# Attention and two gated MLPs: value loads cut to the rows that are read

## The chip, the cores and the metric

The program runs on one core of one Trainium2 chip. A core has TensorE (PE in the profile, its weight loads PEld), VectorE (DVE), ScalarE (ACT), GpSimd (POOL), SyncE (SP), and 16 DMA engines that move data between HBM and SBUF. The metric is the device time of one execution in microseconds, median of several runs.

## The reference

```python
q, k, v: (4 batches, 8 heads, 576 tokens, 64)          # attention
q_d, k_d, v_d = mean over groups of 4 tokens            # 144 pooled tokens
out_d = softmax(scale * q_d @ k_d.T) @ v_d              # pooled attention
out_up = repeat(out_d, 4, axis=tokens)
mask = |i - j| < 4                                      # local attention: a band of 7 keys
out_local = softmax(where(mask, scale * q @ k.T, -1e9)) @ v
x = (out_up + out_local) as (2304 tokens, 512)
x = (sigmoid(x @ w_gate) * (x @ w_val)) @ w_out         # first MLP, inner width 1536
h = x @ w_in;  x = (h * sigmoid(1.702 * h)) @ w_out     # second MLP, inner width 2048
```

All in float32.

## The kernel before

The 32 pairs of batch and head are worked through as 16 units of two heads. After the units the two MLPs run as a long row of 128x128 by 128x384 matmuls (lines 662 to 664, 653 and 808 to 810).

**Local attention of a unit.** The 576 queries are cut into 12 windows of 48. A window needs 56 keys (four more on each side). `weigh(u)` (L615) multiplies, for each window and head, the turned probabilities `p_t` by the values `vw`: 57 rows, the 56 keys and one row that carries a small constant for the sum of probabilities. Head 0 stands in partitions 0 to 56, head 1 in partitions 64 to 120; rows 57 to 63 and 121 to 127 of `vw` are loaded and never read. One row of `vw` is 12 windows of 65 numbers, 3120 bytes.

**Pooled attention of a unit.** `sum_values(u)` (L556) adds values over groups of four tokens with five matmuls of 128 tokens each (`vt`, 5 chunks of 128 columns, two heads side by side). 576 tokens fill four chunks and 64 rows of the fifth; the other 64 rows of the fifth come from HBM as zeros. One row of `vt` is 2560 bytes. `sum_values_1` (L567) is the same for unit 1 in another bank.

**The loads.** All are issued by SP in one program order. `load_q` and `load_k` have four buffers, `load_vt` and `load_vw` two. `load_vw(u)` (L348) waits until `weigh(u - 2)` is over, `load_vt(u)` (L343) until the pooled scores of unit u - 2 are made. Ahead of the loop stand, in this order, q and k of unit 0, `vt` 0, q and k of 1, `vw` 0, `vt` 1, q and k of 2, `vw` 1, q and k of 3. In the loop (L453) step i issues `vw` i + 2, q and k of i + 6, `vt` i + 4, and in ten of the steps a half of an MLP weight block (`load_in_half`, `load_out_half`), 256 KB. Each load raises its semaphore by 16 when it has landed.

**PE's order.** In the loop (L876) PE runs for unit i: `weigh(i)`, the mask of i + 2, `turn(i + 1)`, `score(i + 2)`, `turn_out(i)`, `weigh_pooled(i)`, `sum_values(i + 2)`, `score_pooled(i + 2)`, `turn_pooled(i + 1)`. Nothing is reordered at run time: an instruction that waits holds all behind it. Between `weigh(14)` and `weigh(15)` the first products of the MLP stand (L889 to L894).

**Ahead of it all** DVE clears constants and pads; its last one, `p_t`, raises `zeroed` (L1587), for which PE waits ahead of `sum_values(0)`, and the casts of `picks` and `mask` come after.

Of the kernel before, what the change touches and what calls it, by code (L numbers as in the profile page):

```python
# [14 lines left out]
B, H, S, D = 4, 8, 576, 64  # L15
FACTOR = 4
P = 128
# [10 lines left out]
KW = QW + 2 * PAD  # L28
# [3 lines left out]
HK = 64  # L32
SD = S // FACTOR
SD1 = SD - P
VT = 5
HQ = SD // 2
VC = D + 1
SCALE = 1.0 / D ** 0.5
# [92 lines left out]
def attention_mlp_kernel(nc, q_t, k_t, v_win, v_tok, w_gate_val, w_out1, w_in2, w_out2, out):  # L131
    with ExitStack() as ctx:
        top = [16512]

        def place(name, shape, dtype=F32, at=None):
            size = 2 if dtype == BF16 else 4
            for s in shape[1:]:
                size *= s
            where = top[0] if at is None else at
            if at is None:  # L140
                top[0] += (size + 31) // 32 * 32
            return nc.alloc_sbuf_tensor_at(name, shape, dtype, offset=where)
# [4 lines left out]
        def sems(name, n):  # L147
            return [sem(f"{name}{i}") for i in range(n)]
# [16 lines left out]
        w = [place(f"w{i}", [P, 2, NP, WG], F32R) for i in range(2)]  # L165
# [17 lines left out]
        vw = [place(f"vw{i}", [P, NWIN, VC]) for i in range(2)]  # L183
        vt = [place(f"vt{i}", [P, VT, P]) for i in range(2)]
        e = place("e", [P, PAIRS, 2, HK])
        p_t = place("p_t", [P, NWIN, HK])
        o_tok = place("o_tok", [P, PAIRS, 2, D])
        pd = [place(f"pd{i}", [HQ, 4, SD]) for i in range(2)]
        pd_t = place("pd_t", [P, 2, 2, SD])
# [55 lines left out]
        vw_loaded = sems("vw_loaded", 2)  # L245
        vt_loaded = sems("vt_loaded", 2)
# [76 lines left out]
        def _(sp):  # L323
# [19 lines left out]
            def load_vt(u):  # L343
                if u >= 2:
                    sp.wait_ge(scored_d, u - 1)
                sp.dma_start(vt[u % 2][:, :, :].rearrange("p j d -> p (j d)"), v_tok[u]).then_inc(vt_loaded[u % 2], 16)

            def load_vw(u):  # L348
                if u >= 2:
                    sp.wait_ge(weighed, u - 1)  # L350
                sp.dma_start(vw[u % 2][:, :, :].rearrange("p w d -> p (w d)"), v_win[u]).then_inc(vw_loaded[u % 2], 16)

            def load_in(b):

# [89 lines left out]

            load_qk(0)
            load_vt(0)
            load_qk(1)
            load_vw(0)
            load_vt(1)
            load_qk(2)  # L450
            load_vw(1)
            load_qk(3)
            for i in range(-2, UNITS - 2):  # L453
                if i >= 0:
                    load_vw(i + 2)
                if i + 6 < UNITS:
                    load_qk(i + 6)
                if i + 4 < UNITS:
                    load_vt(i + 4)
                if i in (-1, 0):  # L460
                    load_in_half(0, i + 1)
                if i in (1, 2):
                    load_in_half(1, i - 1)
                if i in (3, 4):
                    load_out_half(0, i - 3)
                if i in (8, 9):
                    if i == 8:
                        sp.wait_ge(wa_ready, 1)
                        sp.wait_ge(wsum_ready, 1)
                    load_in_half(2, i - 8)  # L470
                if i in (10, 11):
                    load_out_half(1, i - 10)
# [61 lines left out]
        def _(pe):  # L534
# [20 lines left out]

            def sum_values(u):  # L556

                pe.wait_ge(vt_loaded[u % 2], 16 * (u // 2) + 16)
                if u >= 2:
                    pe.wait_ge(exped_d, u)  # L560
                    pe.wait_ge(v_summed, u)
                for j in (0, 2, 1, 3, 4):
                    bank, at = divmod(j // 2 * 64, P)
                    pe.matmul(d_ps[at:at + 64, bank, VS_AT:VS_AT + P], fours[:, j % 2, :], vt[u % 2][:, j, :],
                              start=(j % 2 == 0), stop=(j % 2 == 1 or j == VT - 1))

            def sum_values_1():  # L567

                pe.wait_ge(vt_loaded[1], 16)
                for j in (0, 2, 1, 3, 4):  # L570
                    c, at = divmod(j // 2 * 64, P)
                    mm = pe.matmul(t_ps[at:at + 64, 1, VS1_AT + c * P:VS1_AT + (c + 1) * P], fours[:, j % 2, :], vt[1][:, j, :],
                                   start=(j % 2 == 0), stop=(j % 2 == 1 or j == VT - 1))
                mm.then_inc(sums_turned, 1)

            def score_pooled(u):
# [4 lines left out]
                for half in range(2):  # L581
                    for h in range(2):
                        rows = slice(h * D, (h + 1) * D)
                        mm = pe.matmul(d_ps[0:HQ, h, half * SD:(half + 1) * SD],
                                       qkd[u % 2][rows, 0, half * HQ:(half + 1) * HQ], qkd[u % 2][rows, 1, :],
                                       start=True, stop=True)
# [13 lines left out]
            def turn_pooled(u):  # L600
# [6 lines left out]
                for c, keys in enumerate((slice(0, P), slice(P, SD))):  # L607
                    for h in range(2):
                        for half in range(2):
                            at = c * SD + half * HQ  # L610
                            mm = pe.transpose(t_ps[0:keys.stop - keys.start, h, at:at + HQ],
                                              pd[u % 2][:, 2 * h + half, keys], ident[0:HQ, 0:HQ])
                mm.then_inc(turned_d, 1)

            def weigh(u):  # L615

                pe.wait_ge(copied, u + 1)
                pe.wait_ge(vw_loaded[u % 2], 16 * (u // 2) + 16)
                if u >= 1:
                    pe.wait_ge(added, u)  # L620
                for pair in range(PAIRS):
                    for par in range(2):
                        w = 2 * pair + par
                        for h in range(2):
                            rows = slice(HK * h, HK * h + KW + 1)
                            mm = pe.matmul(o_ps[HK * par:HK * (par + 1), h, pair * VC:(pair + 1) * VC],  # L626
                                           p_t[rows, w, :], vw[u % 2][rows, w, :], start=True, stop=True)
                mm.then_inc(weighed, 1)
# [226 lines left out]
            pe.wait_ge(fours_step, 3)  # L855
            pe.wait_ge(zeroed, 1)
            sum_values(0)
            score_pooled(0)
            masks(1)
            score(1)  # L860
            pe.wait_ge(ident_ready, 1)
            turn(0)
            sum_values_1()
            score_pooled(1)
            weigh(0)
            masks(2)
            turn_pooled(0)
            score(2)
            turn_out(0)
            turn(1)  # L870
            sum_values(2)
            weigh_pooled(0)
            score_pooled(2)
            turn_pooled(1)
            last = UNITS - 1
            for i in range(1, UNITS - 2):  # L876
                weigh(i)
                masks(i + 2)
                turn(i + 1)
                score(i + 2)  # L880
                turn_out(i)
                weigh_pooled(i)
                sum_values(i + 2)
                score_pooled(i + 2)
                turn_pooled(i + 1)
            weigh(last - 1)
            turn(last)
            pe.wait_ge(shifted, UNITS)
# [624 lines left out]
        def _(dve):  # L1513
            vec = nc.vector
# [67 lines left out]
                vec.memset(qk[slot][:, 1, PAD + S:S + 2 * PAD], 0.0)  # L1582
            vec.memset(e[:, :, :, KW:KW + 1], 1.0)
            vec.memset(e[:, :, :, KW + 1:HK], 0.0)
            vec.memset(d_ps[:, 1, VS_AT:VS_AT + P], 0.0)
            vec.memset(t_ps[:, 1, VS1_AT:VS1_AT + 2 * P], 0.0)
            vec.memset(p_t[:, :, QW:HK], 1.0).then_inc(zeroed, 1)  # L1587
# [3 lines left out]
            for half in range(2):  # L1591
                rows = slice(HK * half, HK * half + HK)
# [4 lines left out]
            for half in range(2):  # L1597
                rows = slice(HK * half, HK * half + QW)
# [801 lines left out]
```

## Time and profile before

| | us |
|---|---|
| median of 3 runs | 871.63 (871.37 to 872.4) |
| the profiled execution, its own time | 872.51 |
| its span in the profile | 870.8 |
| PE busy in it | 857.5 |
| DVE, ACT, POOL busy | 624.1, 487.0, 589.2 |
| last `weigh` starts | 109.67 |

The span runs from the first instruction to the last; the 1.7 us around it belong to start and end of the execution. In the timeline a row is: start in us, duration in us, engine, line, operation, tiles (output <- inputs), shapes and how many instructions were merged; in brackets the idle time ahead of it and what ended that. A line such as L626 is a line of the kernel printed above. The attention is about the first eighth of the span, the MLPs all the rest.

### The profile page before, as it was taken

Reading aid. Unit: us, or ns where it says so; the run is one execution under the profiler, and the core shown is the slowest. Engines: PE = TensorE matmul, PEld = TensorE weight load, DVE = VectorE, ACT = ScalarE, POOL = GpSimd, SP = SyncE. Lnnn points to the kernel's source line nnn. Section 1 sums busy time; section 2 is a strip of 40 time slices with the busy share of each in tenths; the row PEclk is TensorE's granted clock in tenths of the full one; section 3 lists DMA queues with packets and bytes.
Section 4 is the critical chain, followed back from the end, with each engine's and each line's share of the span. In section 5 each row is a group of like instructions: output and inputs, shape, how many; then the busy total and the mean of one; then the engine's idle time right before and its main releaser. Section 6 shows DMA issues by size and latency. Waiting matters only on the chain.

```text
span 870.8 us, 18384 instructions
## 1 busy us (share of the span) xinstructions
PE 857.5 (98%) x6638; PEld 832.2 (96%) x6638; DVE 624.1 (72%) x1140; ACT 487.0 (56%) x1083; POOL 589.2 (68%) x471
## 2 busy tenths in 40 slices
PE   8989999999999999999999999999999999999998
PEld 6878899999999999999999999999999999999998
DVE  5767645555658685967676877777888778878777
ACT  5778754545536364645354646654676466556652
POOL 6688788888758648785457776763668644846523
PEclk9999999999999999999999999999999999999999
DMA  9877466685955787838588825345246751636432
GB/s 329 264 211 218 166 242 237 223 342 204 382 172 192 294 287 292 301 109 285 210 274 305 285 91 205 97 147 195 67 174 218 266 183 59 218 123 230 171 120 73
DMA packets 77369, 184.26 MB, mean 212 GB/s; under 512 B 5856, under 2 KB 31456, under 8 KB 74464
## 3 DMA queue, kind: packets, MB, share of 16 engines
q1 hardware_dynamic: 77280, 183.10, 60.2%
q8 instruction: 53, 0.87, 0.4%
q14 instruction: 36, 0.29, 0.1%
HBM read 141.66 MB, written 41.42 MB: 210 GB/s over the span
## 4 chain that ended last, share of the span: by engine, by line
PE 94%; issue 2%; DVE 1%; ACT 1%; POOL 1%; DMA 1%; SPq 0%; ACTq 0%; DVEq 0%
PE o_ps L808 10%; PE o_ps L809 10%; PE o_ps L810 10%; PE d_ps L662 7%; PE d_ps L664 7%; PE d_ps L663 7%; PE s_ps L662 6%; PE o_ps L653 6%; PE s_ps L664 6%; PE s_ps L663 6%; PE t_ps L662 3%; PE t_ps L663 3%; PE t_ps L664 3%; PE o_ps L626 2%; PE t_ps L597 1%
## 5 line engine op out<-in xcount | busy, mean ns | idle before, releaser
L808 PE MATMUL o_ps<-g_hi,v 128*128 128x384 f32 x504 | 169.6, 337 | 0.6 <-DVE att L1773 0.5
L809 PE MATMUL o_ps<-g_lo,v 128*128 128x384 f32 x504 | 169.4, 336 | 0.0
L810 PE MATMUL o_ps<-g_hi,v 128*128 128x384 f32 x504 | 169.4, 336 | 0.0
L1773 DVE TENSOR_TENSOR att<-o_ps,att 128x384 f32<-128x384 f32 x212 | 118.1, 557 | 56.4 <-PE o_ps L810 53.8
L2123 POOL TENSOR_TENSOR v<-v_f,v 128x512 fp32r<-128x512 f32 x72 | 95.0, 1340 | 56.2 <-ACT v L1076 56.2
L2123 POOL TENSOR_TENSOR v<-raw,v 128x512 fp32r<-128x512 f32 x54 | 70.9, 1312 | 89.8 <-ACT v L1069 77.2
L662 PE MATMUL d_ps<-xs_hi,w 128*128 128x384 f32 x360 | 121.0, 336 | 2.0 <-issue 1.2
L664 PE MATMUL d_ps<-xs_hi,w 128*128 128x384 f32 x360 | 120.5, 335 | 0.0
L663 PE MATMUL d_ps<-xs_lo,w 128*128 128x384 f32 x360 | 120.4, 335 | 0.0
L662 PE MATMUL s_ps<-xs_hi,w 128*128 128x384 f32 x300 | 101.2, 337 | 1.3 <-POOL xs_lo L2153 1.3
L664 PE MATMUL s_ps<-xs_hi,w 128*128 128x384 f32 x300 | 100.5, 335 | 0.0
L663 PE MATMUL s_ps<-xs_lo,w 128*128 128x384 f32 x300 | 100.4, 335 | 0.0
L808 PEld LDWEIGHTS o_ps<-g_hi,v 128*128 128x128 f32 x504 | 94.6, 188 | 1.8 <-issue 1.8
L809 PEld LDWEIGHTS o_ps<-g_lo,v 128*128 128x128 f32 x504 | 94.8, 188 | 0.0
L810 PEld LDWEIGHTS o_ps<-g_hi,v 128*128 128x128 f32 x504 | 94.6, 188 | 0.0
L1191 ACT CAST g_hi<-t_ps 128x384 fp32r<-128x384 f32 x96 | 46.2, 481 | 84.8 <-DVE t_ps L1701 45.0
L662 PEld LDWEIGHTS d_ps<-xs_hi,w 128*128 128x128 f32 x360 | 67.6, 188 | 3.9 <-issue 3.4
L1645 DVE TENSOR_TENSOR g_lo<-g_f,g_hi 128x384 fp32r<-128x384 f32 x68 | 62.1, 914 | 7.9 <-ACT g_hi L1174 7.9
L663 PEld LDWEIGHTS d_ps<-xs_lo,w 128*128 128x128 f32 x360 | 67.6, 188 | 0.0
L664 PEld LDWEIGHTS d_ps<-xs_hi,w 128*128 128x128 f32 x360 | 67.6, 188 | 0.0
L2153 POOL TENSOR_TENSOR xs_lo<-xs_sum,xs_hi 128x768 fp32r<-128x768 f32 x24 | 46.9, 1965 | 26.1 <-ACT xs_hi L1040 26.0
L662 PE MATMUL t_ps<-xs_hi,w 128*128 128x384 f32 x180 | 60.4, 335 | 0.0
(186 smaller groups left out, 2099.6 us busy)
## 6 DMA issues: line engine op xcount, KB each, us to landing
w<-w_split SPq DMA_DIRECT2D x48, 768.0 KB, 7.0
w<-w_split SPq DMA_DIRECT2D x48, 512.0 KB, 7.8
w<-w_split SPq DMA_DIRECT2D x96, 256.0 KB, 5.3
w_split<-w SPq DMA_DIRECT2D x12, 1792.0 KB, 6.7
raw<-in_w_out_dram SPq DMA_DIRECT2D x36, 512.0 KB, 4.5
w_split<-job_w SPq DMA_DIRECT2D x8, 1792.0 KB, 7.7
vw<-in_v_win_dram SPq DMA_DIRECT2D x16, 390.0 KB, 4.6
raw<-in_w_gate_val_dram SPq DMA_DIRECT2D x24, 256.0 KB, 3.3
```

The source lines that it names most:

```text
L653: mm = pe.matmul(bank, a, b, start=(i == 0), stop=(i == len(steps) - 1))
L662: pe.matmul(bank, wh[:, cols], xh[:, c, :], start=(start and c == 0), stop=False, skip_group_check=True)
L663: pe.matmul(bank, wh[:, cols], xl[:, c, :], start=False, stop=False, skip_group_check=True)
L664: mm = pe.matmul(bank, wl[:, cols], xh[:, c, :], start=False, stop=(c == 1), skip_group_check=True)
L808: pe.matmul(bank, vh, gh, start=(start and k == c), stop=False, skip_group_check=True)
L809: pe.matmul(bank, vh, gl, start=False, stop=False, skip_group_check=True)
L810: mm = pe.matmul(bank, vl, gh, start=False, stop=(k == c + 1), skip_group_check=True)
L1191: nc.scalar.copy(g_hi[k % 2][:, t, :], bank[LAST[k] % 2]).then_inc(thi_ready[t], 1)
L1645: vec.tensor_tensor(g_lo[k % 2][:, PIECE[n], :], gated_at(k, n, bank), g_hi[k % 2][:, PIECE[n], :], ALU.subtract).then_inc(g_ready[n], 1)
L1773: vec.tensor_tensor(part, value, part, ALU.add).then_inc(y_added, 1)
L2123: gp.tensor_tensor(v_all[:, :, 1, v_part, :], source, v_all[:, :, 0, v_part, :], ALU.subtract).then_inc(vp_ready, 1)
L2153: gp.tensor_tensor(xs_lo[at][:, :, :], source, xs_hi[at][:, :, :], ALU.subtract).then_inc(x_ready, 1)
```

## The change

The load of `vw` becomes two, of rows 0 to 56 and 64 to 120. The load of `vt` becomes two: four chunks of all 128 rows (2048 bytes a row), and the fifth chunk of 64 rows (512 bytes a row). The other half of the fifth chunk is cleared once by DVE in both buffers. The semaphores now rise by 32 for each unit, and the waits count so.

```diff
+V_END = S - (VT - 1) * P
...
             def load_vt(u):
                 if u >= 2:
                     sp.wait_ge(scored_d, u - 1)
-                sp.dma_start(vt[u % 2][:, :, :].rearrange("p j d -> p (j d)"), v_tok[u]).then_inc(vt_loaded[u % 2], 16)
+                sp.dma_start(vt[u % 2][:, 0:VT - 1, :].rearrange("p j d -> p (j d)"), v_tok[u][:, 0:(VT - 1) * P]).then_inc(vt_loaded[u % 2], 16)
+                sp.dma_start(vt[u % 2][0:V_END, VT - 1, :], v_tok[u][0:V_END, (VT - 1) * P:VT * P]).then_inc(vt_loaded[u % 2], 16)
 
             def load_vw(u):
                 if u >= 2:
                     sp.wait_ge(weighed, u - 1)
-                sp.dma_start(vw[u % 2][:, :, :].rearrange("p w d -> p (w d)"), v_win[u]).then_inc(vw_loaded[u % 2], 16)
+                for h in range(2):
+                    rows = slice(HK * h, HK * h + KW + 1)
+                    sp.dma_start(vw[u % 2][rows, :, :].rearrange("p w d -> p (w d)"), v_win[u][rows, :]).then_inc(vw_loaded[u % 2], 16)
...
-                pe.wait_ge(vt_loaded[u % 2], 16 * (u // 2) + 16)
+                pe.wait_ge(vt_loaded[u % 2], 32 * (u // 2) + 32)
...
-                pe.wait_ge(vt_loaded[1], 16)
+                pe.wait_ge(vt_loaded[1], 32)
...
-                pe.wait_ge(vw_loaded[u % 2], 16 * (u // 2) + 16)
+                pe.wait_ge(vw_loaded[u % 2], 32 * (u // 2) + 32)
...
             vec.memset(e[:, :, :, KW + 1:HK], 0.0)
+            for i in range(2):
+                vec.memset(vt[i][V_END:P, VT - 1, :], 0.0)
             vec.memset(d_ps[:, 1, VS_AT:VS_AT + P], 0.0)
```

SP's queue ahead of the loop, before. The number after a tile's name is a buffer, and rows x columns stand last.

```order
L346 DMA vt_87<-in_v_tok_dram 128x640
L331 DMA qk_82<-in_q_t_dram 128x576
L337 DMA qk_82<-in_k_t_dram 128x576
L351 DMA vw_85<-in_v_win_dram 128x780
L346 DMA vt_88<-in_v_tok_dram 128x640
```

The same place now:

```order
L347 DMA vt_87<-in_v_tok_dram 128x512
L348 DMA vt_87<-in_v_tok_dram 64x128
L332 DMA qk_82<-in_q_t_dram 128x576
L338 DMA qk_82<-in_k_t_dram 128x576
L355 DMA vw_85<-in_v_win_dram 57x780 x2
L347 DMA vt_88<-in_v_tok_dram 128x512
L348 DMA vt_88<-in_v_tok_dram 64x128
```

Nothing changes places; `vt` and `vw` are now two issues each, in the places of the one. In the kernel before every load has 128 rows; the two of `vw` now have 57 and the second of `vt` has 64.

## Rows read from the trace of the kernel before

**Rows 1.** The page, busy time of each engine over the span.

```profile
PE 857.5 (98%) x6638; PEld 832.2 (96%) x6638; DVE 624.1 (72%) x1140; ACT 487.0 (56%) x1083; POOL 589.2 (68%) x471
```

**Rows 2.** DMA packets, and all issues: tiles, queue, count, KB each, us to landing.

```profile
DMA packets 77369, 184.26 MB, mean 212 GB/s; under 512 B 5856, under 2 KB 31456, under 8 KB 74464
...
w<-w_split SPq DMA_DIRECT2D x48, 768.0 KB, 7.0
w<-w_split SPq DMA_DIRECT2D x48, 512.0 KB, 7.8
w<-w_split SPq DMA_DIRECT2D x96, 256.0 KB, 5.3
w_split<-w SPq DMA_DIRECT2D x12, 1792.0 KB, 6.7
raw<-in_w_out_dram SPq DMA_DIRECT2D x36, 512.0 KB, 4.5
w_split<-job_w SPq DMA_DIRECT2D x8, 1792.0 KB, 7.7
vw<-in_v_win_dram SPq DMA_DIRECT2D x16, 390.0 KB, 4.6
raw<-in_w_gate_val_dram SPq DMA_DIRECT2D x24, 256.0 KB, 3.3
vt<-in_v_tok_dram SPq DMA_DIRECT2D x16, 320.0 KB, 4.5
qk<-in_q_t_dram SPq DMA_DIRECT2D x16, 288.0 KB, 3.5
qk<-in_k_t_dram SPq DMA_DIRECT2D x16, 288.0 KB, 4.0
job_raw<-in_w_in_dram SPq DMA_DIRECT2D x8, 512.0 KB, 8.8
v_f<-in_w_out_dram SPq DMA_DIRECT2D x12, 256.0 KB, 7.0
out_dram<-att SPq DMA_DIRECT2D x2, 1536.0 KB, 12.6
out_dram<-att SPq DMA_DIRECT2D x8, 192.0 KB, 1.9
```

**Rows 3.** Windows: us, busy of each engine (instructions), granted clock, DMA share, GB/s.

```profile
7.50:10.90 3.40, 3.40 (x65) 2.50 (x62) 0.75 (x1) 1.07 (x5) 1.81 (x2) 0.54 1.03 398
44.00:50.00 6.00, 3.70 (x115) 2.96 (x114) 2.10 (x4) 3.87 (x14) 3.86 (x5) 1.00 0.66 215
```

**Rows 4.** Timeline of PE in the attention, some of its rows.

```profile
6.92 1.26 PE L564 MATMUL d_ps<-vt,fours 128*64 128x128 f32 x10 [1.65 <-DMA vt<-in_v_tok_dram]
...
17.28 0.87 PE L564 MATMUL d_ps<-vt,fours 128*64 128x128 f32 x10
...
49.59 0.41 PE L551 MATMUL s_ps<-qk 64*48 64x56 f32 x13 [2.30 <-issue]
...
59.37 0.93 PE L626 MATMUL o_ps<-vw,p_t 57*64 57x65 f32 x48
...
65.41 0.93 PE L626 MATMUL o_ps<-vw,p_t 57*64 57x65 f32 x48
...
71.45 0.93 PE L626 MATMUL o_ps<-vw,p_t 57*64 57x65 f32 x48
...
101.83 0.93 PE L626 MATMUL o_ps<-vw,p_t 57*64 57x65 f32 x48
...
109.67 0.93 PE L626 MATMUL o_ps<-vw,p_t 57*64 57x65 f32 x48
```

**Rows 5.** Timeline of SP's queue: the first load, and one of `vw`.

```profile
0.80 0.39 SPq L331 DMA_DIRECT2D qk<-in_q_t_dram  x1
...
60.36 0.33 SPq L351 DMA_DIRECT2D vw<-in_v_win_dram  x1
```

**Rows 6.** Timeline of DVE at the start: a clear of 128x128.

```profile
1.52 0.17 DVE L1585 MEMSET d_ps<- 128x128 f32 x1
```

## The prediction

> **What bounds the kernel now.** I read the busy line of the page first, then TensorE's timeline in the attention, then the DMA parts and the windows. The busy line has PE at 857.5 us of a span of 870.8 [rows 1], so any time in which PE stands longer is added to the end nearly one for one. In the attention one unit follows the other at the pace of PE: `weigh` starts at 59.37, 65.41 and 71.45, 6.04 us a unit, with no idle time ahead of it, and the two last start at 101.83 and 109.67, with MLP products between them [rows 4]. Values are waited for in one place, at the start: `sum_values(0)` stands 1.65 us for `vt` [rows 4]. The loads run far ahead: `vw` of unit 9 is issued at 60.36 [rows 5] and read at 71.45 [rows 4], and such a load lands 4.6 us after its issue [rows 2]. So there is little to win from fewer bytes, and about 11 us of lead to lose per unit before PE notices. The question is what the new shapes do to the DMA engines.
>
> **The bytes.** `vw` goes from 128 to 114 rows, 390 to 347 KB; `vt` from 320 to 288 KB. That is 75 of 1286 KB for a unit (q and k are 576 of it) [rows 2], 6%.
>
> **How a load is spread, the term that decides.** All issues of the kernel sum to 366 (the 15 kinds), and there are 5856 packets under 512 B [rows 2]; 5856 / 366 is 16.0. No data row of before is that short (the shortest piece is 1 KB), so these are the completion marks, one for each of 16 engines: each load, always of 128 rows, is split over all 16, 8 rows each. No load of another count is in the trace. 57 is 3 x 19. If a load is split into equal shares over at most 16 engines, which is all that rows 2 show, 57 rows go over 3 engines (or one), 19 rows each; 64 rows go over 16. If the shares may be unequal, 57 rows go four to an engine, over 15. I take the equal split over 3, and the same 3 for both halves.
> The Trainium skill, "DMA: Bandwidth & Descriptors", section "Why a DMA increments its semaphore by 16 and not by 1", has it as a rule: the number of engines is the largest up to 16 that divides the row counts of both sides, with 100 rows on 10 engines as an example, and always the lowest-numbered ones. No row of before can test it, since 128 gives 16.
>
> **What the three engines then carry.** When all are busy (share 1.03) they move 398 GB/s, 24.9 GB/s each [rows 3]. At that rate, for an engine among the three:
> - q and k of a unit: 16 rows of 2304 bytes, 1.48 us
> - `vt`: 8 rows of 2048 and 4 of 512 bytes, 0.74 us (before, 8 rows of 2560: 0.82)
> - `vw`: 2 x 19 rows of 3120 bytes, 118.6 KB, 4.76 us (before, 8 rows: 1.00)
> - a half block of MLP weights, 256 KB over 16: 0.66 us, in ten of the units.
> Sum 6.98 us a unit, 7.64 with a half block; before it was 3.30 and 3.96. Both new ones are above PE's 6.04. The three engines become the bound of the attention, and since the lead of 11 us is finite, PE stands at `weigh` in nearly each unit.
>
> **The sum.** Engine 0 to the end of `vw` 14, whose loads are issued behind q, k and `vt` of all 16 units and all ten half blocks: 16 x 1.48 = 23.7, 16 x 0.74 = 11.8, 15 x 4.76 = 71.4, 10 x 0.66 = 6.6, together 113.5 us. It is not idle on the way: at first it has a backlog, and later each `weigh` waits for it while the next `vw` is already queued. Ahead of that stands the first issue at 0.80 [rows 5], and the fixed part of a load, 3.5 us to landing of an early q less 0.74 us of moving [rows 2], 2.8 us. So `vw` 14 lands at 117.1. `weigh(14)` started at 101.83: 15.3 us later. From there to `weigh(15)` PE has 7.8 us of other work and `vw` 15 comes 4.8 us behind `vw` 14, hidden. That is the lower figure, at the best rate. Packets in a less tidy queue, and the start, where the engines are not yet full, cost some per cent: with 3% on 113.5 it is 18.7. I take 17.5. The profiled execution took 872.51, 0.9 over the median of 871.63; on it the sum gives 890.0, on the median 889.1. I say 889.5, 2.1% slower.
> Bounds for the price of a row of `vw` on one engine: 125 ns from the full rate [rows 3]; from above, (4.6 - 2.8) us / 8 rows = 0.23 us, from the median landing with all that stands ahead of it in the queue [rows 2]. By that a unit has 8.7 us for `vw` alone and `vw` 14 comes 59 us later still. A queue that never empties is the case of [rows 3], so I stay near the first.
>
> **The same at the start.** `vt` 2 is behind `vw` 0 and `vw` 1 on the three engines: 5 pairs of q and k 7.4, three `vt` 2.2, two `vw` 9.5, sum 19.1 us, landing at 22.7. PE wants it at 17.28 [rows 4], so `sum_values(2)` stands some 5 us. This is not added to the sum: the engines work through it, and it is the first part of the same 17.5.
>
> **The small parts.** SP issues 32 loads more. An issue takes 0.33 us in the loop [rows 5], two more per 6.04 us, and SP waits there most of the time: 0. Ahead of the loop four more issues stand, 0.4 us each [rows 5], before q and k of unit 3; behind the DMA backlog: 0 (at most 1.6 us, if there were none). DVE's two clears of 64x128 take about 0.17 us each, as the 128x128 one [rows 6], ahead of the casts that PE's first scores wait for. It costs nothing as long as PE waits for `vt` 0 until 6.92 with 1.65 us to spare [rows 4], else 0.34 us. PE's matmuls are the same.
>
> **The rivals.**
> - Unequal shares, or other engines for each load in turn. Then an engine carries no more than the 8 rows of `vw` for a unit that it carried before, on average, so 3.2 to 3.9 us, under 6.04, and the lead hides all: 871.6, at most a few tenths less for the 32 KB taken from `vt` 0. For it speaks only that rows 2 show nothing but 128 rows.
> - The clock comes on top. PE ran at half (mean 0.54) in 7.50 to 10.90 [rows 3] after it had stood 1.65 us, having run for few us before. There five-chunk sums take 1.26 us and not 0.87 [rows 4]; by 1.45 a unit takes 8.8 us, above 7.6, and PE itself becomes the bound where that happens. If half of 14 units run so, 7 x (8.8 - 7.3) = 10 us more: 900. Against it: at 49.59 PE had stood 2.30 us [rows 4], and the clock of that stretch is 1.00 [rows 3]; the waits I expect are 0.9 to 1.6 us. One early fall behind the 5 us stand is likely, and hidden by the engines' backlog.
> - One engine, the other equal split: 114 x 0.125 + 2.2 = 16.5 us a unit, 1030 us or so.
> - Faster. With all 16 engines in use, `vt` 0 could come early enough that PE doesn't stand at 6.92 and keeps its clock. That is 1.65 us, and about 1.1 us for the 3.4 us at half clock (3.4 - 3.4 / 1.45): 868.9. It decides only if `vt` 0 lands 1.6 us earlier; ahead of and in it 864 KB stand in place of 896, 0.1 us at 398 GB/s. So hardly.
>
> **How the numbers follow.** Three engines, 879 to 900: 0.74. With the clock or dearer packets, above that: 0.09, and one engine 0.01. Unequal shares, no change: 0.12. Faster by the start: 0.04. No change means within 0.2%, 1.7 us, about what a measurement of this kernel can tell. Slower has the first three, 0.84. The range from 879 to 906 holds the three-engine case with the bottom at 6 us of regained time (PE's later idle, shorter packets than I took) and most of the clock's; it leaves out 0.2.
>
> **What would show it.** Right: packets in the two halves of `vw` from 3 engines, so a mean DMA share in the attention that falls while PE stands; `vw` landing 7 us or more after its issue; waits of PE for a DMA at L630 (the former L626) of about 1 us in some ten units; `weigh` 7.0 to 7.7 us apart; a stand of about 5 us at the third `sum_values`; the last `weigh` near 127; the MLPs as long as before. Wrong: `weigh` still 6.04 us apart and `vw` landing in under 5 us, which is the split over all 16; or PE rows of 1.26 us for five chunks in the middle of the attention, which is the clock.

## The result: 3.3% slower

| | before | after |
|---|---|---|
| median of 6 runs, us | 870.96 | 899.51 |
| lowest and highest | 870.29, 872.40 | 896.39, 903.17 |
| profiled execution, its own time | 872.51 | 896.39 |
| span in the profile | 870.8 | 894.6 |

The ratio after to before is 1.0328, with a 95% interval of 1.0311 to 1.0345. I had forecast 889.5 us, 2.1% slower, with 879 to 906 as the range. The direction and the mechanism came out; the loss is 28.5 us between the medians and not 18. The profiled execution is the fastest of the six, 23.9 us over the one of before; what follows explains those 23.9.

**All of it is in the attention.** Windows of PE for the MLPs alone, from 17.3 us behind the start of the last `weigh` to the end; first the kernel before, then the one after. The columns are those of [rows 3].

```profile
127.00:870.80 743.80, 736.87 (x4218) 732.13 (x4216) 542.17 (x972) 399.12 (x810) 493.90 (x359) 1.00 0.59 208
```

```profile
150.70:894.60 743.90, 737.10 (x4218) 732.49 (x4217) 540.84 (x972) 399.73 (x810) 494.55 (x359) 1.00 0.59 208
```

The same work takes 743.8 and 743.9 us. So the 23.8 us of the span lie ahead of it.

**Three engines.** The page after, the line of the DMA packets, against the first of [rows 2]:

```profile
DMA packets 78265, 183.04 MB, mean 205 GB/s; under 512 B 5952, under 2 KB 32576, under 8 KB 75360
```

Packets under 512 B are the completion marks (the shortest data rows are 512 B). Of the 366 loads of before the 16 of `vw` are gone and 16 second loads of `vt` are new: again 366 loads with 16 marks, 5856. The 96 that are left over are 32 loads of 57 rows with 3 marks each. The split is the equal one, over 3 engines.

The trace's packet records, which give start, duration and size of each packet but not its engine, bear this out in two ways. While rows of `vw` move, the kernel after has mostly three of them under way at once (three for 60 us, more for 6 us), so both loads of a unit use the same three engines. And of all data packets, fewer than three are under way for only 0.1 us between 2.5 and 124.9 us, exactly three for 42 us; in the kernel before fewer than three are under way for 9.4 us between 2.5 and 100 us. So the three engines work through without a pause.

**PE waits for it.** The timeline of PE after, its `weigh` rows in the attention and the stands at the start (answers to [rows 4]; L630 is the former L626, L576 and L568 the former L572 and L564):

```profile
15.28 1.54 PE L576 MATMUL t_ps<-vt,fours 128*64 128x128 f32 x10 [4.90 <-DMA vt<-in_v_tok_dram]
...
17.92 1.58 PE L630 MATMUL o_ps<-vw,p_t 57*64 57x65 f32 x48
...
26.84 0.76 PE L568 MATMUL d_ps<-vt,fours 128*64 128x128 f32 x9 [2.15 <-DMA vt<-in_v_tok_dram]
...
30.96 0.93 PE L630 MATMUL o_ps<-vw,p_t 57*64 57x65 f32 x48
...
51.18 1.40 PE L630 MATMUL o_ps<-vw,p_t 57*64 57x65 f32 x48 [1.54 <-issue]
...
74.80 1.17 PE L630 MATMUL o_ps<-vw,p_t 57*64 57x65 f32 x48 [1.70 <-issue]
...
82.33 0.93 PE L630 MATMUL o_ps<-vw,p_t 57*64 57x65 f32 x48
...
90.08 0.93 PE L630 MATMUL o_ps<-vw,p_t 57*64 57x65 f32 x48 [1.63 <-issue]
...
97.73 0.93 PE L630 MATMUL o_ps<-vw,p_t 57*64 57x65 f32 x48 [1.53 <-issue]
...
106.03 0.93 PE L630 MATMUL o_ps<-vw,p_t 57*64 57x65 f32 x48 [0.65 <-issue]
...
114.34 0.93 PE L630 MATMUL o_ps<-vw,p_t 57*64 57x65 f32 x48 [2.20 <-issue]
...
126.58 0.93 PE L630 MATMUL o_ps<-vw,p_t 57*64 57x65 f32 x48
...
133.39 0.93 PE L630 MATMUL o_ps<-vw,p_t 57*64 57x65 f32 x48
```

Unit 1 starts at 30.96 where it started at 20.34. Units 3 to 12 are 7.5 to 8.3 us apart and not 6.04. The last two start at 126.58 and 133.39, against 101.83 and 109.67 in [rows 4]: 24.8 and 23.7 us later. The profile calls the wait ahead of `weigh` "issue" here. That it is the wait for `vw` is seen in the packet records: in the six units where PE stood, `weigh` starts 0.3 to 0.9 us after the last row of its `vw` is in. In e7, where that wait stands alone and last ahead of `weigh`, the profile names the loads (below).

The page has PE busy for 867.7 us, 10.2 more than in [rows 1], though its matmuls are the same: in parts of the attention they ran at a lower clock. The other 13.6 of the 23.8 us are idle time. Whether the lower clock made the end later is another question; e7 takes it up.

SP's queue shows the other side of it. In these rows of SP after, an issue that mostly takes 0.33 us in the loop of before [rows 5] takes up to 2.92 us (the second row is two issues): SP stands in the issue itself. In the kernel before the longest issue of q, k or `vw` took 1.26 us.

```profile
8.29 2.92 SPq L332 DMA_DIRECT2D qk<-in_q_t_dram  x1
...
20.33 3.03 SPq L355 DMA_DIRECT2D vw<-in_v_win_dram  x2
...
47.14 2.58 SPq L338 DMA_DIRECT2D qk<-in_k_t_dram  x1
```

The loads land late. `vw` 5 is issued at 44.50 and its last row is in at 58.44, 13.9 us later, where the median was 4.6 in [rows 2]. k, 4.0 us from issue to landing in [rows 2], takes 11.9. That it waits for its rows behind `vw` on the three engines is argued; the records name no engine.

```profile
qk<-in_k_t_dram SPq DMA_DIRECT2D x16, 288.0 KB, 11.9
```

### The profile page after: what moved, and what is told of

Same layout as the page of the kernel before. It is cut to its first block, busy times and chain, and to the rows that moved or that the text cites. A ratio compares the mean times of both kernels' runs of the same rounds, so it can differ in the third digit from the quotient of the medians.

```text
span 894.6 us, 18418 instructions
## 1 busy us (share of the span) xinstructions
PE 867.7 (97%) x6638; PEld 840.4 (94%) x6638; DVE 623.0 (70%) x1142; ACT 488.5 (55%) x1083; POOL 590.0 (66%) x471
## 2 busy tenths in 40 slices
DMA packets 78265, 183.04 MB, mean 205 GB/s; under 512 B 5952, under 2 KB 32576, under 8 KB 75360
## 4 chain that ended last, share of the span: by engine, by line
PE 92%; issue 2%; DMA 1%; SPq 1%; DVE 1%; POOL 1%; ACT 1%; ACTq 0%; DVEq 0%
PE o_ps L812 10%; PE o_ps L814 10%; PE o_ps L813 10%; PE d_ps L666 7%; PE d_ps L668 7%; PE d_ps L667 7%; PE s_ps L666 6%; PE o_ps L657 6%; PE s_ps L668 6%; PE s_ps L667 6%; PE t_ps L666 3%; PE t_ps L668 3%; PE t_ps L667 3%; PE o_ps L630 2%; PE t_ps L601 1%
```

## The experiments

The ratios are of means, not of the medians given beside them; they stand against runs of the kernel before on the same chip, with their 95% interval. The mean time of a packet of 3120 bytes (one row of `vw`) is from the trace's packet records; it was 165 ns before (most 124, the first ones of a burst far more) and is 138 ns after.

**e1: the split of `vt` alone.** The changed kernel with

```diff
-                for h in range(2):
-                    rows = slice(HK * h, HK * h + KW + 1)
-                    sp.dma_start(vw[u % 2][rows, :, :].rearrange(...), v_win[u][rows, :]).then_inc(vw_loaded[u % 2], 16)
+                sp.dma_start(vw[u % 2][:, :, :].rearrange(...), v_win[u]).then_inc(vw_loaded[u % 2], 16)
```

and the count of 16 in `weigh`.

> vt in two loads (128 rows of 2048 bytes, 64 rows of 512) with the cleared half chunk, vw in one load of 128 rows as before. Theory A (the loss is the two loads of 57 rows, which go over 3 of 16 engines, 19 rows of 3120 bytes each): no change, 870 to 872 us, PE stands only for vt 0 at the start, 6112 short packets (16 for each of 382 loads). Theory B (the loss comes from more issues on SP and from short rows): slower, by about a third of the 28.5 us, 878 or more.

870.53 us, ratio 1.0002 (0.9991 to 1.0012), 6112 short packets. The second load of `vt`, its short rows, the issues and the two clears cost nothing that can be measured.

**e2: the split of `vw` alone.** The kernel before with the two loads of 57 rows.

> vw in two loads of 57 rows, vt in one load as before. Theory A: the whole loss, 896 to 902 us; a unit of the three engines takes 4.76 + 1.48 + 0.82 = 7.06 us and 7.72 with a half block. Short packets 5856 - 16 x 16 + 32 x 3 = 5696. Theory B: two thirds of the loss, about 890.

900.13 us, ratio 1.0342 (1.0320 to 1.0363), the whole loss. Short packets 5697, one more than foreseen.

**e3: two loads of 64 rows.** The kernel before, `vw` in its lower and its upper half:

```diff
+                for h in range(2):
+                    rows = slice(HK * h, HK * h + HK)
```

> vw in two loads of 64 rows (all rows, as before), vt in one load. As many issues and waits as with 57 rows and more bytes, but 64 is 16 x 4. Theory A: no change, 870 to 872 us. A rival, that two loads of disjoint halves go one behind the other and each pays its fixed time: landing 2 us later, still inside the lead of 11 us, but PE stands longer at the start: 873 to 876.

874.07 us, ratio 1.0053 (1.0030 to 1.0075). Not the 3.3% of 57 rows: two issues, two landings and more bytes than these cost a sixth of it. But it isn't nothing: theory A had said 870 to 872, and the figure lies in the range of its rival. e9 takes that up.

**e4, e6, e5 and e10: the count of rows, with bytes nearly the same.** The changed kernel, one number edited:

```diff
-                    rows = slice(HK * h, HK * h + KW + 1)
+                    rows = slice(HK * h, HK * h + 60)       # e4; 58 in e5, 59 in e10, + KW (56) in e6
```

In e6 the 57th row, the same in all units, is loaded in two loads of one row for each of the two buffers, once, so that nothing is loaded that isn't read.

> As the changed kernel, with 60 rows in each load of vw and not 57: 5% more bytes, but 60 is 15 x 4. Theory A: 15 engines carry 8 rows each, no change from before, 870 to 872 us, short packets 5856 + 256 - 256 + 32 x 15 = 6336. If the loss had to do with rows beside the 64-row halves, or with partitions that start at 64, it would stay at 896 to 902.

> The changed kernel with the loads of vw cut at 56 rows (14 x 4, 14 engines), the 57th row, which is the same for all units, loaded once into each buffer. Fewer bytes than any other form and no row that isn't read. Equal split: short packets 5856 + 256 - 256 + 32 x 14 + 4 = 6308, the attention as long as before. As in e3 and e4 each load writes to one half of the partitions, so at the start the rows are dear: 871 to 874 us, not faster than before.

> As the changed kernel, one row more in each load of vw: 58 is 2 x 29, so 2 engines with 29 rows each. Equal split: vw takes 2 x 29 x 3120 bytes = 7.27 us on each of the two, a unit 9.5 us (10.1 with a half block), vw 14 at 0.8 + 2.8 + 151 = 155 us, and with the 9 us that three engines lost beyond the sum 164: 925 to 934 us, short packets 5856 + 256 - 256 + 32 x 2 = 5920. If what costs is the number of loads or rows that are no power of two, it stays near 900.

> As the changed kernel with 59 rows in each load of vw. 59 is prime: one engine with 118 rows, 14.8 us at 24.9 GB/s, 17.0 us a unit (17.6 with a half block). vw 14 at 0.8 + 2.8 + 263 = 267 us, and with the 9 us lost beyond the sum so far 276: 1036 to 1048 us, short packets 5856 + 256 - 256 + 32 = 5888.

| rows in a load | short packets | engines by that | rows per engine and unit | median us | ratio (interval) |
|---|---|---|---|---|---|
| 60 (e4) | 6336 | 15 | 8 | 872.57 | 1.0021 (1.0005 to 1.0037) |
| 56 (e6) | 6308 | 14 | 8 | 871.99 | 1.0008 (0.9993 to 1.0022) |
| 57 (after) | 5952 | 3 | 38 | 899.51 | 1.0328 (1.0311 to 1.0345) |
| 58 (e5) | 5920 | 2 | 58 | 934.05 | 1.0719 (1.0697 to 1.0740) |
| 59 (e10) | 5888 | 1 | 118 | 1052.06 | 1.2073 (1.2048 to 1.2097) |

One row less than 57 or three more, and the loss is gone or nearly so (the 0.2% of e4 is just clear of the noise); one or two more, and it doubles or grows sixfold. The number of engines is the divisor each time. The packet records agree: rows of `vw` are mostly under way two at a time in e5 (two for 96 us, more for 6) and singly in e10 (one for 234 us, two for 7.5), and between 2.5 and 270 us there is never a moment in e10 without a data packet. e10 came 4 us above my figure: `vw` 15 lands 15 us behind `vw` 14, and PE has only 7.8 us of other work between the two, so the last `weigh` waits as well. Its timeline of PE has the two last, of which the second is 177.7 us later than in [rows 4]:

```profile
272.30 1.58 PE L630 MATMUL o_ps<-vw,p_t 57*64 57x65 f32 x48 [8.19 <-issue]
...
287.38 1.58 PE L630 MATMUL o_ps<-vw,p_t 57*64 57x65 f32 x48 [6.11 <-issue]
```

**e7: does the clock make the loss larger?** The changed kernel, with small matmuls ahead of PE's wait for `vw`; that wait is moved behind the one for `added`:

```diff
-                pe.wait_ge(vw_loaded[u % 2], 32 * (u // 2) + 32)
                 if u >= 1:
                     pe.wait_ge(added, u)
+                if 2 <= u < UNITS - 2:
+                    for _ in range(FILL):                   # 14
+                        pe.matmul(o_ps[:, 1, PAIRS * VC:PAIRS * VC + 120], warm[:, 0:P], warm[:, 0:120], start=True, stop=True)
+                pe.wait_ge(vw_loaded[u % 2], 32 * (u // 2) + 32)
```

> The changed kernel with 14 small bf16 matmuls (120 columns, into a part of o_ps that nobody reads) ahead of PE's wait for vw in units 2 to 13, some 0.7 us of work that stands where PE waits anyway. Theory C (the 10 us over my forecast are the half clock that follows each stand of PE): the clock stays up in the middle of the attention and the time falls by 3 to 8 us, to 891 to 896. Theory D (the three engines set the pace whatever PE does): 898 to 902, the waits ahead of weigh shorter by what the fillers take.

899.25 us, ratio 1.0320 (1.0296 to 1.0345): as the changed kernel. The middle of the attention in e7 (the granted clock stands ahead of the DMA share):

```profile
45.00:60.00 15.00, 12.72 (x266) 10.44 (x264) 8.64 (x16) 9.10 (x30) 8.99 (x13) 1.00 0.54 169
60.00:75.00 15.00, 14.80 (x314) 12.38 (x315) 9.16 (x18) 9.00 (x29) 10.29 (x11) 0.89 0.54 168
75.00:90.00 15.00, 12.30 (x298) 10.20 (x297) 8.04 (x16) 9.72 (x32) 9.84 (x12) 1.00 0.49 158
90.00:105.00 15.00, 12.99 (x293) 10.85 (x290) 7.10 (x15) 8.41 (x31) 8.46 (x9) 0.89 0.64 189
```

In the changed kernel the clock of the same four windows is 0.89, 1.00, 0.89 and 0.89. So the fillers did not keep the clock up: they took away one of three low stretches there. At the start, where no fillers stand, the clock is as low as after (0.66 in 10 to 20 us). One low stretch less is worth about 1 us of PE's work, if it is like the one of [rows 3] (the prediction's own estimate, 3.4 - 3.4 / 1.45), and the four runs of e7 lie 3.9 us apart. The time alone therefore doesn't refute theory C, though the 3 to 8 us that it promised did not come.

The packet records of the changed kernel speak against it more firmly. Up to the last row of `vw` 14 the three engines have no pause (fewer than three packets for 0.1 us), so a slower PE kept none of them waiting; a faster PE would have stood longer ahead of `weigh`. And behind 105 us, where PE sets the pace again, the clock was whole (1.00 in 105 to 135 us). What PE waits for is also named in e7 (us in total, times, longest):

```profile
PE o_ps L634 <- DMA vw<-in_v_win_dram: 8.8, 7, 2.0
```

In the changed kernel it was 9.3 us, 6 times, 2.2 at most, so the waits hardly shrank, where theory D had them shorter by what the fillers take; e7's own rows were dearer (145 ns).

**e8: the first two units whole.**

```diff
+                if u < 2:
+                    sp.dma_start(vw[u][:, :, :].rearrange(...), v_win[u]).then_inc(vw_loaded[u], 32)
+                    return
```

> The changed kernel, but vw of units 0 and 1 comes in one load of 128 rows each, the other 14 units as 2 x 57. The three engines carry 2 x (4.76 - 1.00) = 7.5 us less, all of it ahead of vt 1 and vt 2. Engines set the pace: 7.5 us less at the floor price, 10 at the price that the rows had there (0.17 us each), so 889 to 892. If PE's stands at the start (4.90 and 2.15 us) were a loss of their own on top of the engines' work, some 17 us less: 882.

890.24 us, ratio 1.0201 (1.0164 to 1.0237). That is 9.3 us less than the changed kernel by the medians, 10.7 by the means, in runs made at another time; the four of e8 lie between 885.13 and 890.83. PE's long stands at the start are gone: the waits that the profile gives to `vt` are now 0.9 and 0.4 us. Yet what was gained is what the three engines had less to carry (7.5 us at 125 ns a row, 10 at 0.17 us), not the 17 us that the stands and what follows them look like in the timeline. PE then waits more in the middle, 14.8 us against 9.3:

```profile
PE o_ps L633 <- issue: 14.8, 11, 2.6
```

**e9: the same two loads of 64 rows, by even and odd partitions.**

```diff
+                for h in range(2):
+                    rows = slice(h, P, 2)
```

> vw in two loads of 64 rows as in e3, but one takes the even partitions and the other the odd ones, not the lower and the upper half. Same issues, rows per engine and bytes. Theory P (in e3 16 engines wrote to the 64 partitions of one half, which have half of the SBUF's DMA ports; the rows took 186 ns in the mean, 124 in the best case): the mean price of a row falls under 165 ns and the time to 870 to 872. Theory Q (two loads in place of one cost 0.5% at the start by themselves): 873 to 875, as e3.

871.10 us, ratio 0.9997 (0.9988 to 1.0007), against 1.0053 (1.0030 to 1.0075) of e3. The mean row took 158 ns, 186 in e3; half of the rows took over 158 in e3, and in e9 three of four took 124. The same number of loads and issues, with as many rows each: only the partitions of a load differ. So it isn't the second load that cost the 0.5%. The Trainium skill, "SBUF — State Buffer", section "Door 1: The DMA port swizzle (why `[64,N]` ≈ `[32,N]`)", says that partitions 0 to 63 lie on 8 of 16 DMA ports. The runs agree with that (186 and 158 ns a row), but no record here names a port. The profiled run of e3 is the fastest of its five (872.48 us), so its trace shows the dearer rows and not the 0.5%.

## Why the prediction was right, and where its size was off

- **How a load is spread.** Right: 5952 short packets, 32 x 3 of them for the halves of `vw`. That 5856 / 366 is 16 was the only trace of it in the kernel before; e5 and e10 show the rule at 2 and 1, e6 and e4 at 14 and 15.
- **The three engines become the bound.** Right: `weigh` 7.5 to 8.3 us apart in the middle, where I had said 7.0 to 7.7; six waits of 0.65 to 2.20 us ahead of it, 9.3 us in all, where I had said some ten of about 1 us; and the time follows what the busiest engine carries, in e5, e8 and e10.
- **The small parts at nothing.** Right: e1, and for a second load of `vw` in itself e9.
- **The sum, and the term that was too small: the price of a row, 125 ns "at the best rate".** I took `vw` for 15 units as 71.4 us of an engine's time. The packet records have 79.0 (15 x 114 rows / 3, mean 139 ns): 7.6 us more. 3.5 of these are in units 0 and 1, whose rows took 168 and 173 ns while the first loads still ran on all engines; from unit 3 on a row took 124 to 144 ns. The last row of `vw` 14 ended at 124.9, where I had its landing at 117.1: 7.8 us later. `weigh(14)` came 1.7 us after that, at 126.58. It did not wait for `vw` 14: PE's last wait was for unit 12 (2.20 us, at 114.34), and two units of PE's own work followed. The sum at 139 ns gives 15.3 + 7.6 + 1.7 = 24.6 us for `weigh(14)`, and 24.8 was measured. My ends for the price were 0.125 and 0.23 us; I took the lower one, and 13% of the way up was right.
- **Two smaller errors in that sum cancel, and that is luck.** I began the engines' work at 3.6 us, with the whole fixed part of a load ahead of it. The first data packet starts at 2.1 us, 1.5 earlier. From there to 124.9 the three engines worked 122.7 us each, 43.7 of them for all but `vw`, where I had 42.1: 1.6 more.
- **3% for a less tidy queue.** This was the allowance that stood for that price, 3.4 us on 113.5, and I then took 17.5 and not the 18.7 that it gave. 7.6 us were needed, over 10% of the rows' time.
- **The stand at the start.** I had about 5 us at the third `sum_values`, for `vt` 2. It came at the second, 4.90 us for `vt` 1, and 2.15 at the third. `vt` 1 stands behind `vw` 0 only, but it is wanted first. That it isn't added to the rest was right, and e8 shows it.
- **The clock.** It fell where I gave it 9%: 0.69 and 0.67 in 10 to 30 us, three times 0.89 later. The rival on the clock gave 900 us, almost the 899.5 that was measured, but not for its reason: the three engines have no pause that a slower PE could have made (under e7), so the clock had no price of its own up to `vw` 14. e7's time by itself can't tell, since one low stretch of three went.

What stays open: the account above explains 23.9 us and not 28.5. The median of the six runs lies 3.1 us above the profiled one, and the profiled one of before 1.5 us above its own median. e2 and e7 with the same loads had rows of 143 and 145 ns in their profiles: the price of a row seems to differ from run to run, and why wasn't tried. Nor is it shown why rows on three engines cost more than 125 ns. Other loads that write to the same DMA ports are a candidate after e3 and e9, not more.

## What to carry to other kernels

Ahead of a cut of a load to the rows that are read, divide the row count by the numbers up to 16: what counts is rows times bytes on the busiest engine, per turn of the loop, against the time of a turn. A slow load holds up all that stands behind it on its engines, and a lead of 11 us only decides when that is seen. A profile of the new kernel can show the split: here the packets under 512 B gave the number of engines of each load. Cut to 56 or 60 rows, or load 128: the 6% of bytes saved here bought nothing in any form (e1, e4, e6); by the sum of the prediction no engine was short of time before.

## What the runs showed of the hardware

- Each load tried was split over the largest number of engines up to 16 that divides its rows: marks for 16, 15, 14, 3, 2 and 1 engines at 128 or 64, 60, 56, 57, 58 and 59 rows.
- Two loads of 64 rows, one for each half of the partitions, were dearer than two of 64 rows in every other partition: 186 and 158 ns a row of 3120 bytes, 874.07 and 871.10 us.
- SP stood up to 2.92 us in one issue that mostly takes 0.33 us in the kernel before, where 1.26 us was the most. That it waits for the engines of the earlier loads is argued, not shown.
- PE's granted clock fell to its lower level (1.2 GHz) shortly after stands of 1.54, 1.70 and 1.53 us ahead of `weigh`: mean 0.53 in 51.20 to 54.60, 0.58 in 74.80 to 78.90 and 0.56 in 98.80 to 102.70. It stayed at the full 2.4 GHz after stands of 1.63 us at 90.08 (1.00 in 90.10 to 97.00) and 2.20 us at 114.34 (1.00 in 105 to 120), and after one of 2.30 us in the kernel before [rows 3, 4]. So the length of the last stand alone doesn't decide it.
